# Load order, wait placement and the routing's token tables in a fused RWKV attention, mixture-of-experts and MLP kernel

## What is computed

```python
# 1: recurrent attention, B, H, S, D = 2, 8, 768, 48
for t in range(S):
    cur = einsum('bhd,bhe->bhde', u * k_t, v_t)
    y[:, :, t] = einsum('bhd,bhde->bhe', r_t, state + cur)
    state = w[..., None] * state + einsum('bhd,bhe->bhde', k_t, v_t)
# 2: x = y as (1536, 384); 8 experts, capacity 384 each, first come first served
logits = x @ w_gate; e = argmax(logits); gate = softmax(logits)[e]
out[i] = gate[i] * (relu(x[i] @ w1[e]) @ w2[e])     # 0 where the expert is full
# 3: an MLP, 384 -> 2048 -> 384
h = relu(out @ w_in); result = (h * h) @ w_out
```

## Time and profile before

| | |
|---|---|
| median of 3 runs | 427.11 us (426.66 to 428.65) |
| the profiled execution's own time | 429.13 us |
| its span, first to last instruction | 427.4 us |
| PE busy | 409.7 us (96%) |
| DVE / ACT / POOL busy | 260.0 / 217.4 / 67.5 us |
| moved by DMA | 66.02 MB |

### The profile page before, as it was taken

The page is one execution under the profiler, slowest core; times in us unless marked ns, Lnnn a source line. Parts: engine busy times, 40 slices in busy tenths (PEclk is TensorE's granted clock), DMA queues, the critical chain, the costliest instruction groups (busy, mean ns, idle before and its releaser), DMA issues.

```text
span 427.4 us, 10156 instructions
## 1 busy us (share of the span) xinstructions
PE 409.7 (96%) x3969; PEld 377.4 (88%) x3969; DVE 260.0 (61%) x452; ACT 217.4 (51%) x430; POOL 67.5 (16%) x76
## 2 busy tenths in 40 slices
PE   8699996899999999999999999999999999999994
PEld 4599995599999999999998899899889988998984
DVE  6469688777786766677747553556465446535331
ACT  4567788155555564655536444444445355444321
POOL 3545651640201202000000000004000004000003
PEclk9889999699999999999999999999999999999999
DMA  7999984299646656545562232235223224200002
GB/s 206 232 251 261 266 298 147 97 320 397 234 165 245 213 162 234 197 173 195 184 212 75 84 136 79 74 99 192 79 74 124 97 74 142 80 2 0 0 2 81
DMA packets 18734, 66.02 MB, mean 154 GB/s; under 512 B 2888, under 2 KB 7641, under 8 KB 18704
## 3 DMA queue, kind: packets, MB, share of 16 engines
q1 hardware_dynamic: 16912, 60.93, 44.8%
q0 software_dynamic: 1792, 4.72, 3.0%
HBM read 59.35 MB, written 7.08 MB: 155 GB/s over the span
## 4 chain that ended last, share of the span: by engine, by line
PE 77%; DVE 4%; issue 1%; ACT 1%; POOL 0%; DVEq 0%; ACTq 0%; POOLq 0%
PE score_banks L601 19%; PE y_banks L601 18%; PE spare_bank L624 6%; PE gate_bank L624 6%; PE state_bank L624 6%; PE sum_bank L624 6%; PE sum_bank L614 5%; PE state_bank L614 5%; PE gate_bank L614 5%; PE spare_bank L558 1%; PE spare_bank L591 1%; DVE hlo L1140 0%; ACT cv L787 0%; DVE onehb L1060 0%; DVE onehb L1117 0%
## 5 line engine op out<-in xcount | busy, mean ns | idle before, releaser
L949 DVE TENSOR_TENSOR wlo<-raw,whi 128x1536 fp32r<-128x1536 f32 x56 | 98.3, 1757 | 90.8 <-ACT whi L746 87.6
L746 ACT ACTIVATE whi<-raw 128x1536 fp32r<-128x1536 f32 x56 | 83.3, 1489 | 83.0 <-PE spare_bank L624 46.8
L467 POOL DMA_INDIRECT out<-osb,oidx x12 | 12.9, 1072 | 247.4 <-ACT osb L891 244.4
L1136 DVE TENSOR_TENSOR sq<-rl 128x512 f32<-128x512 f32 x48 | 32.9, 688 | 29.8 <-ACT rl L833 29.8
L436 POOL DMA_INDIRECT xg<-attention_out,gidx x16 | 20.3, 1268 | 68.7 <-PE spare_bank L591 63.0
L1140 DVE TENSOR_TENSOR hlo<-sq,hhi 128x512 fp32r<-128x512 f32 x48 | 30.9, 685 | 0.0
L601 PE MATMUL y_banks<-yhi,whi 128*128 (+1 forms) x72 | 28.5, 395 | 0.0
L601 PE MATMUL score_banks<-yhi,wlo 128*128 (+1 forms) x72 | 28.4, 395 | 0.0
L601 PE MATMUL y_banks<-yhi,wlo 128*128 (+1 forms) x72 | 28.4, 395 | 0.0
L601 PE MATMUL score_banks<-yhi,whi 128*128 (+1 forms) x72 | 28.4, 394 | 0.0
L601 PE MATMUL y_banks<-ylo,whi 128*128 (+1 forms) x72 | 28.4, 394 | 0.0
(11 more groups left out here) (231 smaller groups left out, 1143.3 us busy)
## 6 DMA issues: line engine op xcount, KB each, us to landing
raw<-in_wts SPq DMA_DIRECT2D x56, 768.0 KB, 4.5
tok<-in_tok SPq DMA_DIRECT2D x12, 384.0 KB, 6.7
feat<-in_feat SPq DMA_DIRECT2D x16, 192.0 KB, 5.1
vT<-in_vT SPq DMA_DIRECT2D x12, 192.0 KB, 5.1
attention_out<-x_sb SPq DMA_DIRECT2D x12, 192.0 KB, 5.4
out<-rl SPq DMA_DIRECT2D x12, 192.0 KB
feat<-in_feat SPq DMA_DIRECT2D x4, 448.0 KB, 8.9
xg<-attention_out,gidx POOLq DMA_INDIRECT x16, 4.6
```

Source lines behind the costliest of these rows:

```text
L467: nc.gpsimd.indirect_dma_start(out=out[:, :], out_offset=bass.IndirectOffsetOnAxis(ap=oidx[:, t:t + 1], axis=0), in_=osb[:, t, :], in_offs ...
L746: return nc.scalar.activation(dst, src, ACT.Copy)
L949: v.tensor_tensor(wlo[:, r, :], raw[:, r, :], whi[:, r, :].bitcast(F32), ALU.subtract).then_inc(w_lo, 1)
L1136: v.tensor_tensor(sq[:, ft, :], rl[:, ft, :], rl[:, ft, :], ALU.mult).then_inc(h_sq, 1)
```

## The change

```diff
@@ SP, loads
             load_features(1)
             load_gate_values(1)
             load_tokens(1)
+            sp.wait_ge(state_used, 1)
             load_features(2)
+            load_gate_values(2)
             load_tokens(2)
-            for n in range(NT):
+            for n in range(1, NT):
                 sp.wait_ge(vwg_psum, n + 1)
                 if n + 2 < NT:
                     load_gate_values(n + 2)
-                if n == 0:
+                if n == 1:
                     load_features(3)
-                if n + SLOTS < NT:
-                    sp.wait_ge(decayed, 2 * n + 2)
-                    load_features(n + SLOTS)
-                if n + 3 < NT:
-                    if n:
-                        sp.wait_ge(khat_ready, n)
-                        sp.wait_ge(vx_ready, 2 * n)
-                    load_tokens(n + 3)
-                if n:
-                    sp.wait_ge(x_ready, n)
-                    store_x(n - 1)
+                elif n + 3 < NT:
+                    sp.wait_ge(decayed, 2 * n)
+                    load_features(n + 3)
+                if n + 2 < NT:
+                    if n >= 2:
+                        sp.wait_ge(khat_ready, n - 1)
+                        sp.wait_ge(vx_ready, 2 * n - 3)
+                    load_tokens(n + 2)
+                if n == 1:
+                    sp.wait_ge(decayed, 2)
+                    load_features(4)
+                sp.wait_ge(x_ready, n)
+                store_x(n - 1)
@@ POOL
-                    pool.wait_ge(prod_ready, n - 1)
+                    pool.wait_ge(prod_ready, max(n - 1, 2))
                 nc.gpsimd.tensor_tensor(chunk_view(Kd[b][0:ROWS, :]), ...
-                if n >= 2:
-                    pool.wait_ge(state_used, n - 1)
-                pool.wait_ge(in_vT[b], 16 * (n // 2 + 1))
+                if n == 1:
+                    continue
+                pool.wait_ge(state_used, n - 1)
                 nc.gpsimd.tensor_tensor(chunk_view(Rd[b][0:ROWS, :]), ...
@@ POOL, ahead of the gathers
-            pool.wait_ge(matched, 1)
-            nc.gpsimd.tensor_tensor(tokb[:, :, :, :], match[:, :, :].unsqueeze(2).to_broadcast([P, NT, 2, E * CT]),
-                                    token[:, :, 0:2].unsqueeze(3).to_broadcast([P, NT, 2, E * CT]), ALU.mult).then_inc(tokb_ready, 1)
@@ PE
-            pe.wait_ge(in_vT[0], 16)
             with pe.Fori(0, NT // 2) as i:
                 for b in range(2):
                     n = 2 * i + b
 
                     pe.wait_ge(decayed, 2 * n + 2)
+                    pe.wait_ge(in_vT[b], 16 * (i + 1))
@@ PE, first_rows
-                warm(9)
+                warm(8)
@@ ACT
                 gate_values(n)
+                bonus(n)
                 if n + 1 < NT:
                     copy_values(n + 1)
-                bonus(n)
@@ DVE, chunks
                 keys(n)
+                if n == 0:
+                    dve.wait_ge(in_feat[1], 16)
+                    v.tensor_tensor(chunk_view(Rd[1][w, :]), chunk_view(feat[1][w, 0, :]), T[w, :, 0:C], ALU.mult).then_inc(decayed, 1)
@@ DVE, behind the counts
             v.tensor_copy(peaki[:, :], peak[:, :]).then_inc(count_ready, 1)
+            v.tensor_tensor(tokb[:, :, :, :], match[:, :, :].unsqueeze(2).to_broadcast([P, NT, 2, W_]),
+                            token[:, :, 0:2].unsqueeze(3).to_broadcast([P, NT, 2, W_]), ALU.mult).then_inc(tokb_ready, 1)
             after(v.tensor_tensor(stt8[:, :, :], ...
```

## The result

The changed kernel takes 424.86 us (median of 12 runs, 423.94 to 427.22) against 428.62 for the kernel before (12 runs, 426.66 to 430.28): a ratio of 0.9921, with a 95% interval of 0.9904 to 0.9937, or 3.4 us less (the two medians as they stand differ by 3.8). It is faster, by more than the 0.5% named in the prediction.

What follows compares the result with a forecast made beforehand. PE, busy 96% of the span, bounds the kernel, with time lost in chunks 1 and 2 and DMA the second limit. Attention 4.2 plus tables 0.1 gave 4.3 us off 427.1: 422.8, range 420.8 to 427.2.

Steps and rivals of the forecast that it cites:

- main case: Attention and routing: chunk 3 starts near 23.5 with the stop at 1.5 us or less; 4.3 us gained, 422.8; chance 0.5.
- (b): Chunk 1's L530: PE issues one matmul, then nothing for 2.79 us, read as PE out of instructions.
- (c): Chunk 1 behind the stop: the clock falls to 1.2 GHz, so the rest takes twice as long.
- (a): Chunk 1's start: products are late, POOL makes Kd and Rd one after the other, PE waits until 13.53.
- Rd on DVE: Chunk 1: Rd on DVE beside or behind POOL's Kd starts the chunk 0.6 us earlier (bounds 0 and 1.2).
- The load order: SP's loads: tok 1 still at 13.55, feat 3 at 21.0, chunk 3 at 23.5 instead of 28.13; 4.6 us gained.
- The stop: PE's standstill in chunk 1's L530, 2.79 us before, was allowed at most 1.5 us after the change.
- Does the gain last?: Chunks 4 to 11: late tok 4 loses 0.4 us (0 to 0.9), then loads keep up; attention ends 4.2 earlier.
- ACT's order: ACT's copy of the next chunk's tokens moves behind the bonus, ahead of the state's copies: worth zero.
- The tables: Routing: one-hots 0.96 us earlier, mostly taken back by tokb ahead of PE's branch; 0.1 us gained (-0.3 to +0.96).
- Rival A: Chunk 1's stop stays, its packet perhaps fetched only when PE is there; gain only 0.7 us, 426.4; chance 0.3.
- Rival B: Attention: loads fall behind with the shorter queue, state copies wait behind tok on ACT; slower, 431.1; chance 0.1.

Runs made afterwards that it cites:

- rd_back: Changed kernel with Rd of chunk 1 on POOL again: 425.59 us, 0.9942 of the kernel before.
- short_warmups: Kernel before with 48 warm-up matmuls of 128 columns in place of the first 12 of 512, 72 more instructions ahead of chunk 0: 428.53 us, single run.
- tables_back: Changed kernel with the routing's tables as before (tokb on POOL ahead of the gathers, 9 warm-up matmuls): 425.68 us, 0.9943 of the kernel before.
- vt_back: Changed kernel with the wait for vT on POOL ahead of Rd again and none on PE inside its loop: 424.41 us, 0.9928 of the kernel before.
- act_back: Changed kernel with ACT's old order (next chunk's tokens copied ahead of the bonus): 426.32 us, 0.9957 of the kernel before.
- deep_queue: Changed kernel with feat 2, tok 2, feat 3 and tok 3 issued at once, before the wait for chunk 0: 428.03 us, 0.9992 of the kernel before.
- loads_only: Kernel before with the new load order (SP's part of the diff) alone: 426.5 us, 0.9951 of the kernel before.
- all_but_loads: Changed kernel with SP's load order of before: 428.18 us, 0.9987 of the kernel before.

## Why the prediction was right

The forecast was 422.8 us from a median of 427.11, 4.3 less, with 422 to 424 for the main case. Measured are 424.86, inside the range of 420.8 to 427.2 and above the main case's own. The median of before itself moved to 428.62 with more runs, so that the ratio is the fair reading: 3.4 less, 0.8 of what was forecast. The mechanism of the main case is the one that came about; some of its steps were wrong, and two of them cancelled. By the steps:

- **What bounds the kernel.** Right: the first 30 us gave all of the gain, 5.63 us at chunk 3 in the two traces, and the rest kept its length; of the three places it was (b) and (c), since (a) by itself reaches nothing (`rd_back`). That the stop is PE out of instructions was a reading; `short_warmups` and the times of the packet show it.
- **Rd on DVE.** Chunk 1 starts at 12.57 where 12.9 was forecast; feat 1 landed at 10.79 instead of 11.12. POOL's Kd took 1.73 us beside DVE's Rd, of 0.68: here POOL was the one held up. `rd_back` shows that the edit is worth nothing at chunk 3, as the sum had it. But what chunk 1 gained ended already in chunk 2, which waits 0.52 us for POOL's Rd in the changed kernel, and not in a wait for feat 3. With that wait, chunks 1 and 2 took 9.93 us where the sum had 9.1.
- **The load order.** "Tok 1 lands at 13.55 still" was wrong: it landed at 12.12, though the seven large loads up to it are the same. With it, the rate of 223 KB per us was too low: 276 GB/s between 12 and 24 us instead of 228. So feat 3 was there at 19.0 instead of 21.0, and chunk 3 started at 22.50 instead of 23.5. Part of this is the single execution: in the seven others with the short queue and no stop chunk 3 starts at 22.48 to 23.60.
- **The stop.** Up to 1.5 us were allowed; the trace has none, `tables_back` 0.80. The prediction had no working for this bound.
- **Does the gain last?** Chunk 11 came 5.44 us earlier, not 4.2: tok 4 was in time, since the rate was higher. DMA kept up. The chunks took 4.57 us, not 4.55 (4.52 in `vt_back`). So "zero" for PE's new wait was wrong too, though it never waits at L510 in the trace: by the pairs of chunks it costs 0.09 us a pair.
- **ACT's order: "zero" was wrong.** With the new load order the old order of ACT waits 13.0 us for tokens (`act_back`), the new one 0.4; what this is worth in the medians is not clear of noise. The step looked at where ACT idled in the trace of before, in which tokens came early, and not at where the new order would let it wait. The cost didn't show because the change made both edits together.
- **The tables.** 0.1 forecast, 0.1 measured, but by two misses that cancel. `tokb` on DVE took 0.75 us (0.8 forecast), and from the end of chunk 11 `warm` starts 0.2 later than before (0.4 forecast). The transposes then come 0.5 us earlier, where 0.0 to 0.2 was forecast. But the clock stood at 0.50 through them, from 68 to 77 us, and the six took 1.34 us instead of 0.74. The sum had no term for that.
- **The sum** fits the traces from below (4.3 forecast, 5.1 between the two executions) and the medians from above (3.4). The difference between these two is of the size of the stop that came back in `tables_back`; that it is this in the other runs of the changed kernel is possible, and not shown.

**Rival A** had 0.3. The packet did not start because PE had come to the place: in the changed kernel it runs at 11 to 12, PE gets there at 14.6. What speaks for its reading is left over: with the deep queue the packet starts just before PE stops in four of four traces. The Trainium skill (DMA: Bandwidth & Descriptors, Queues, rings and completion order) says that an engine goes round its queue rows packet by packet. In the runs here the time at which the instruction packet starts moves by 3.3 us between the changed kernel and `deep_queue`, so the measurement decides against the way I had used that page. **Rival B** did not come about in the changed kernel; what it described, tokens late at ACT, is what `act_back` and `loads_only` (13.9 us of waiting in 11 places) show, with ACT's old order.

## What to carry to other kernels

A gap of an engine in the middle of a group that has no wait, put down to "issue", can be its instructions: look for a packet on the instruction queue, and move the code by some tens of instructions to see whether the gap moves with it. The queue depth that hides a load's latency can delay the instruction block, and 2.8 us of stop cost as much again by the clock that fell behind it. Loads in the order of need, a chunk at a time, gave 2.1 us by themselves, and 3.4 with the rest of the change, without a byte less. When loads are put later, go through every in-order engine for the copy that waits for them, and put it behind the work that doesn't.

## What the hardware showed that was not expected

- The same loads up to tok 1 landed sooner with nothing queued behind them until 10.4 us: where ACT's wait shows the landing, it is at 12.07 to 12.22 in five traces with the short queue, and at 12.49 to 13.55 in the four with the deep one. That the loads behind slow the ones ahead is a reading of this.
- When POOL's and DVE's products meet, either can be the one that waits: POOL's Kd 1.73 us beside DVE's Rd of 0.68, where in the earlier trace rows DVE's product took 1.67. DVE's `khat` took 1.33 to 1.57 instead of 0.55 beside a product of POOL, and with it came the chunks of 4.85 us and more that do not wait for tokens.
- The clock in the routing differs from execution to execution with the same code path: the routing took 13.7 us in `vt_back`, 14.3 in the changed kernel, 15.6 in `all_but_loads`, where the clock stood at 0.50 from 75 to 85 us.
